# Nine max jobs a head, key copies in the value phase, and the divides on GpSimd in a pooled-attention and Soft-MoE kernel

## The reference

```python
q_pool = q.reshape(B, H, S // 2, 2, D).mean(axis=3)
scores = scale * np.matmul(q_pool, k.transpose(0, 1, 3, 2))
attn = np.exp(scores - np.max(scores, axis=-1, keepdims=True))
attn = attn / (np.sum(attn, axis=-1, keepdims=True) + 1e-09)
x = np.matmul(attn, v)                    # -> (2304, 512)
logits = x @ phi                          # soft MoE: 8 experts, 4 slots each
# softmax over tokens mixes slot inputs, relu(. @ w1) @ w2, softmax over slots mixes back
h = x2 @ w_in                             # then a feed-forward layer, 2048 wide
out = gate(h) @ w_out                     # gate: 0, (h + 1)**2 / 4 or h
```

## Time and profile before

| what | before |
|---|---|
| median of 3 runs (lowest, highest) | 811.72 us (809.96, 811.73) |
| the profiled execution's own time | 812.67 us |
| its span, first to last instruction | 810.8 us |
| busy: PE, DVE, ACT, POOL | 95%, 68%, 59%, 57% |
| attention stage | first exp at 25 us, last sum at 500 us |
| mean granted TensorE clock | 0.989 of full |

### The profile page before, as it was taken

The page is one execution under the profiler, slowest core; times in us unless marked ns, Lnnn a source line. Parts: engine busy times, 40 slices in busy tenths (PEclk is TensorE's granted clock), DMA queues, the critical chain, the costliest instruction groups (busy, mean ns, idle before and its releaser), DMA issues.

```text
span 810.8 us, 14552 instructions
## 1 busy us (share of the span) xinstructions
PE 768.8 (95%) x5181; PEld 575.6 (71%) x5181; DVE 553.2 (68%) x893; ACT 481.1 (59%) x1008; POOL 459.9 (57%) x373
## 2 busy tenths in 40 slices
PE   5899999999999999999999998989799999999996
PEld 3677777776776877777777766524278888888885
DVE  7687887888878878878878873613376454554552
ACT  3677677677676776776776754401565544545452
POOL 2567677677677676676776775000176444444442
PEclk9999999999999999999999999989899999999999
DMA  2222324324334334234243215569900101101011
GB/s 76 78 63 79 103 78 134 99 78 140 94 84 135 94 97 132 83 106 128 78 136 98 79 30 215 196 237 387 387 15 1 40 2 40 27 13 39 0 40 39
DMA packets 47006, 80.63 MB, mean 99 GB/s; under 512 B 9948, under 2 KB 15964, under 8 KB 46940
## 3 DMA queue, kind: packets, MB, share of 16 engines
q1 hardware_dynamic: 46940, 79.77, 31.2%
HBM read 74.89 MB, written 4.79 MB: 98 GB/s over the span
## 4 chain that ended last, share of the span: by engine, by line
PE 46%; POOL 38%; issue 6%; ACT 3%; DVE 3%; DMA 2%; POOLq 0%; SPq 0%; ACTq 0%; DVEq 0%
POOL p_sum L405 33%; PE ps L733 8%; PE ps L732 8%; PE ps L731 8%; POOL p_sum L402 5%; PE ps L490 4%; PE ps L536 3%; ACT probs L796 3%; PE ps L510 2%; PE ps L512 2%; PE ps L721 2%; PE ps L650 2%; DMA w_in<-in_moe_w_in 2%; PE ps L674 1%; PE ps L592 1%
## 5 line engine op out<-in xcount | busy, mean ns | idle before, releaser
L405 POOL TENSOR_TENSOR p_sum<-p_sum,probs 128x576 f32<-128x576 f32 x192 | 271.5, 1414 | 23.2
L1047 DVE TENSOR_REDUCE mx<-ps 128x2 f32<-128x768 f32 (+2 forms) x256 | 216.3, 895 | 23.0 <-PE ps L490 22.9
L796 ACT ACTIVATE probs<-ps 128x576 f32<-128x576 f32 x288 | 184.9, 644 | 38.2 <-PE ps L512 36.5
L510 PE MATMUL ps<-q_rows,k_rows 128*128 128x288 f32 x576 | 172.2, 314 | 0.8 <-ACT probs L796 0.8
L512 PE MATMUL ps<-q_ext,k_ext 128*128 128x288 f32 x576 | 162.2, 296 | 0.0
L439 POOL TENSOR_TENSOR g_lo<-g_buf,g_hi 128x384 fp32r<-128x384 f32 x96 | 100.1, 1043 | 105.3 <-ACT g_hi L952 105.2
L526 PE MATMUL ps<-probs,v_sb 128*64 128x288 f32 x1152 | 146.8, 409 | 1.4 <-ACT probs L796 1.4
L490 PE MATMUL ps<-k_rows,q_rows 128*128 128x384 f32 (+1 forms) x480 | 134.3, 357 | 6.1 <-DVE q_ext L1030 2.9
L510 PEld LDWEIGHTS ps<-q_rows,k_rows 128*128 128x128 f32 x576 | 108.8, 189 | 23.5 <-ACT probs L796 19.6
L1239 DVE SCALAR_TENSOR_TENSOR v_buf<-u_buf 128x384 f32<-128x384 f32 x96 | 58.5, 609 | 92.9 <-ACT u_buf L945 92.7
L526 PEld LDWEIGHTS ps<-probs,v_sb 128*64 128x64 f32 x1152 | 79.9, 137 | 56.2 <-ACT probs L796 1.9
(11 more groups left out here) (170 smaller groups left out, 894.7 us busy)
## 6 DMA issues: line engine op xcount, KB each, us to landing
pre<-in_moe_w SPq DMA_DIRECT2D x47, 512.0 KB, 4.6
k_raw<-in_k SPq DMA_DIRECT2D x32, 288.0 KB, 4.0
v_sb<-in_v SPq DMA_DIRECT2D x32, 288.0 KB, 2.8
q_raw<-in_q SPq DMA_DIRECT2D x32, 256.0 KB, 3.8
from_x<-in_moe_w SPq DMA_DIRECT2D x9, 512.0 KB, 4.5
out<-o_stage SPq DMA_DIRECT2D x36, 128.0 KB, 2.3
p_inv<-inv_dram SPq DMA_DIRECT2D x62, 72.0 KB, 2.6
staged<-in_moe_w SPq DMA_DIRECT2D x8, 512.0 KB, 6.2
```

Source lines behind the costliest of these rows:

```text
L405: nc.gpsimd.tensor_tensor(total, total, probs[u][:, :], ALU.add).then_inc(probs_added, 1)
L510: pe.matmul(ps[:, b0 + h, 0:HALF], k_rows[n % 2][:, P * u:P * u + P], q_rows[n % 2][:, cols], start=True, stop=False)
L796: nc.scalar.activation(probs[u][:, :].rearrange("p (h c) -> p h c", h=2), ps[:, b0:b0 + 2, 0:HALF], ACT.Exp, scale=SCORE_SCALE).then_inc(e ...
L1047: nc.vector.tensor_reduce(mx[0:w, 2 * j:2 * j + len(chunks)], ps[0:w, b:b + len(chunks), 0:CH], AX.X, ALU.max).then_inc(max_free, 1)
```

## The change

Five things change in the attention stage. (1) The half tile's three chunks become three jobs of one chunk each, in banks 6, 7 and 4, so there are nine jobs, the last beside unit 8; its query tile is padded with zeros to 128, and the tiles `q_rows` and `mx` grow. (2) The three key copies of ACT move out of the exps to the value phase, behind the query copies of the same head, two heads ahead. (3) `prepare(n + 2)` stands first in POOL's head. (4) `divide_x` moves from DVE to POOL, behind `prepare` and for head n - 2, with `x_raw` in two buffers and a separate `x_sum` for the sums; DVE keeps head 30's, and the last head's as before. (5) Waits follow from this: ACT's `read_x` on the product two heads back and on the sums' spreading, SP on the last broadcast and on the product before it overwrites `p_inv`, `row_max` and `turn` on other job counts.

```diff
-    JOBS = (CHUNKS + 1) // 2
+    QF = QT - 1
+    PAIR_JOBS = QF * NC // 2
+    JOBS = PAIR_JOBS + NC
@@ job_chunks, job_bank
-            return [(i, i // NC, i % NC) for i in range(2 * j, min(2 * j + 2, CHUNKS))]
+            if j < PAIR_JOBS:
+                return [(i // NC, i % NC) for i in (2 * j, 2 * j + 1)]
+            return [(QF, j - PAIR_JOBS)]
-            return 6 if j % 2 == 0 else 4 if j < JOBS - 1 else 5
+            return (6, 4, 6, 4, 6, 4, 6, 7, 4)[j]
@@ SP: turn_sums
                 sp.wait_ge(sums_inverted, n + 1)
+                if n > 0:
+                    sp.wait_ge(inverses_back, 32 * n)
...
                 sp.wait_ge(inverses_out, 16 * n + 16)
+                if n > 0:
+                    sp.wait_ge(x_done, n)
@@ POOL
+            def divide_x(n):
+                a = D * (n % 2)
+                pool.wait_ge(x_read, n + 1)
+                pool.wait_ge(inverses_back, 32 * n + 32)
+                pool.wait_ge(probs_added, ADDS * (n + 2))
+                pool.wait_ge(q_pooled, min(n + 5, HEADS))
+                nc.gpsimd.tensor_tensor(x_t[a:a + D, n // 2, 0:HALF], x_raw[n % 2][0:D, :], p_inv[0:D, :],
+                                        ALU.mult).then_inc(x_half, 1)
+                pool.wait_ge(x_half, n + 1)
+                nc.gpsimd.tensor_tensor(x_t[a:a + D, n // 2, HALF:SQ], x_raw[n % 2][D:P, :], p_inv[D:P, :],
+                                        ALU.mult).then_inc(x_done, 1)
+                pool.wait_ge(x_done, n + 1)
+
             def head(n):
                 total = p_sum[:, :]
+                if n + 2 < HEADS:
+                    prepare(n + 2)
+                if n > 1:
+                    divide_x(n - 2)
...
-                    if u == 2 and n + 2 < HEADS:
-                        prepare(n + 2)
@@ PE: turn, row_max, weigh
-                        pe.wait_ge(max_free, JOBS * m - 1)
+                        pe.wait_ge(max_free, JOBS * m - 2)
...
+                    if m > 0:
+                        pe.wait_ge(max_free, JOBS * m - 1)
                     pe.wait_ge(q_pooled, m + 1)
...
-                    pe.wait_ge(max_free, JOBS * m + (j - 1))
+                    pe.wait_ge(max_free, JOBS * m + (j - 1 if j < 7 else j - 2))
...
-                    pe.wait_ge(max_free, JOBS * (n + 1) + (JOBS - 2))
+                    pe.wait_ge(max_free, JOBS * (n + 1) + JOBS)
@@ ACT: read_x
+                if n > 1:
+                    act.wait_ge(x_done, n - 1)
                 if n > 0:
-                    act.wait_ge(x_done, n)
+                    act.wait_ge(sums_spread, 16 * n)
@@ ACT: the heads
-                if m == 0:
-                    for j in range(3):
-                        copy_k(0, j)
+                for j in range(3):
+                    copy_k(m, j)
...
                     exp_unit(n, u)
-                    if n + 1 < HEADS and 2 <= u < 5:
-                        copy_k(n + 1, u - 2)
...
                     copy_q(n + 2)
+                    for j in range(3):
+                        copy_k(n + 2, j)
@@ DVE: prologue and heads
+            nc.vector.memset(q_rows[0][:, SQ:QT * P].bitcast(F32), 0.0)
+            nc.vector.memset(q_rows[1][:, SQ:QT * P].bitcast(F32), 0.0)
...
-                if n > 0:
-                    divide_x(n - 1)
+            divide_x(HEADS - 2)
```

More of the change, by code:

```diff
@@ L70, in soft_moe_chain @@
     STEM = 36864
-    AFT = 66176
+    AFT = 67328
     SLOT_AT = 71680
@@ L81, in soft_moe_chain @@
     p_inv = at("p_inv", [P, HALF], 63232)
-    x_raw = at("x_raw", [P, HALF + QUAD], 64384)
+    x_raw = [at("x_raw0", [P, HALF], 64384), at("x_raw1", [P, HALF], 66176)]
+    x_sum = at("x_sum", [P, QUAD], 65536)
     p_spread = at("p_spread", [D, NT], 66112)
@@ L85, in soft_moe_chain @@
     k_ext = [at(f"k_ext{i}", [P, S], AFT + 9216 + 4 * S * i, F32R) for i in range(2)]
[L86 to L91, removed]
+    q_rows = [at(f"q_rows{i}", [P, QT * P], AFT + 18432 + 4 * QT * P * i, F32R) for i in range(2)]
+    q_ext = [at(f"q_ext{i}", [P, QT * P], AFT + 23552 + 4 * QT * P * i, F32R) for i in range(2)]
+    p_sum = at("p_sum", [P, SQ], AFT + 28672)
+    k_raw = at("k_raw", [P, NT, D], AFT + 30976)
+    q_raw = at("q_raw", [P, QT, 2 * D], AFT + 33280)
+    q_pool = at("q_pool", [P, QT, D], AFT + 35840)
     x_nat = at("x_nat", [P, QT, DM], STEM)
@@ L137, in soft_moe_chain @@
     small = {}
-    for name, n in (("ident", P), ("phi_sb", KD * SLOTS), ("sum_ident", SLOTS), ("fold", P), ("mx", 2 * JOBS),
+    for name, n in (("ident", P), ("phi_sb", KD * SLOTS), ("sum_ident", SLOTS), ("fold", P), ("mx", QT * NC),
                     ("neg_max", QT), ("ones", D), ("eps", 1), ("half", 1), ("l_top", 2 * B), ("l_neg", B), ("all_neg", 1),
@@ L169, in soft_moe_chain @@
         scores_ready, exp_done, pv_done = sem("scores_ready"), sem("exp_done"), sem("pv_done")
-        x_read, x_done = sem("x_read"), sem("x_done")
+        x_read, x_half, x_done, x_last = sem("x_read"), sem("x_half"), sem("x_done"), sem("x_last")
         sums_spread, sums_inverted = sem("sums_spread"), sem("sums_inverted")
@@ L297, in turn_sums @@
                 sp.dma_start(p_spread[:, :],
-                             x_raw[0:P:SLOTS, HALF:HALF + QUAD].rearrange("c (p j) -> c p j", j=NT)).then_inc(sums_spread, 16)
+                             x_sum[0:P:SLOTS, :].rearrange("c (p j) -> c p j", j=NT)).then_inc(sums_spread, 16)
                 sp.wait_ge(sums_inverted, n + 1)
+                if n > 0:
+                    sp.wait_ge(inverses_back, 32 * n)
                 sp.dma_start(inv_dram.rearrange("o (p j) -> (o p) j", p=D), p_spread[:, :]).then_inc(inverses_out, 16)
                 sp.wait_ge(inverses_out, 16 * n + 16)
+                if n > 0:
+                    sp.wait_ge(x_done, n)
                 for h in range(2):
@@ L486, in row_max @@
                 else:
-                    pe.wait_ge(max_free, JOBS * m + (j - 1))
-                for b, (i, t, c) in enumerate(job_chunks(j)):
-                    c0, w = q_cols(t)
-                    mm = pe.matmul(ps[0:w, job_bank(j) + b, 0:CH], q_rows[m % 2][:, c0:c0 + w],
+                    pe.wait_ge(max_free, JOBS * m + (j - 1 if j < 7 else j - 2))
+                for b, (t, c) in enumerate(job_chunks(j)):
+                    mm = pe.matmul(ps[:, job_bank(j) + b, 0:CH], q_rows[m % 2][:, P * t:P * t + P],
                                    k_rows[m % 2][:, CH * c:CH * c + CH], start=True, stop=True)
@@ L570, in logits @@
             def logits(b):
-                pe.wait_ge(x_done, 2 * PAIRS * (b + 1))
+                if b < B - 1:
+                    pe.wait_ge(x_done, 2 * PAIRS * (b + 1))
+                else:
+                    pe.wait_ge(x_done, HEADS - 2)
+                    pe.wait_ge(x_last, 2)
                 if b >= 2:
@@ L604, in slot_sums @@
                 if b == 0:
-                    pe.wait_ge(x_done, HEADS)
+                    pe.wait_ge(x_last, 2)
                 else:
@@ L799, in read_x @@
             def read_x(n):
+                if n > 1:
+                    act.wait_ge(x_done, n - 1)
                 if n > 0:
-                    act.wait_ge(x_done, n)
+                    act.wait_ge(sums_spread, 16 * n)
                 act.wait_ge(sums_done, n + 1)
-                nc.scalar.activation(x_raw[:, 0:HALF], ps[:, 4, 0:HALF], ACT.Copy)
-                nc.scalar.activation(x_raw[:, HALF:HALF + QUAD], ps[:, 4, HALF:HALF + QUAD], ACT.Identity,
+                nc.scalar.activation(x_raw[n % 2][:, :], ps[:, 4, 0:HALF], ACT.Copy)
+                nc.scalar.activation(x_sum[:, :], ps[:, 4, HALF:HALF + QUAD], ACT.Identity,
                                      bias=eps[:, :]).then_inc(x_read, 1)
@@ L1043, in top_of_rows @@
             def top_of_rows(m, j):
-                chunks = job_chunks(j)
-                w, b = q_cols(chunks[0][1])[1], job_bank(j)
+                (t, c), n, b = job_chunks(j)[0], len(job_chunks(j)), job_bank(j)
+                w = q_cols(t)[1]
                 dve.wait_ge(max_full, JOBS * m + j + 1)
-                nc.vector.tensor_reduce(mx[0:w, 2 * j:2 * j + len(chunks)], ps[0:w, b:b + len(chunks), 0:CH], AX.X,
+                nc.vector.tensor_reduce(mx[0:w, NC * t + c:NC * t + c + n], ps[0:w, b:b + n, 0:CH], AX.X,
                                         ALU.max).then_inc(max_free, 1)
@@ L1053, in join_tops @@
                     dve.wait_ge(neg_full, m)
-                nc.vector.tensor_reduce(neg_max[:, :], mx[:, 0:CHUNKS].rearrange("p (t c) -> p t c", c=NC), AX.X, ALU.max,
+                nc.vector.tensor_reduce(neg_max[:, :], mx[:, :].rearrange("p (t c) -> p t c", c=NC), AX.X, ALU.max,
                                         negate=True).then_inc(neg_max_ready, 1)
@@ L1072, in divide_x @@
                     last = nc.vector.tensor_tensor(x_t[a:a + D, n // 2, HALF * h:HALF * h + HALF],
-                                                   x_raw[D * h:D * h + D, 0:HALF], p_inv[D * h:D * h + D, :], ALU.mult)
-                last.then_inc(x_done, 1)
```

(4 more changed lines are left out.)

1 line of the change is left out of this document (removed).

## The result

The changed kernel takes 802.13 us (median of 4 runs, 801.74 to 802.85) against 811.73 for the kernel before beside it. The ratio is 0.9888, its 95% interval 0.9871 to 0.9905: faster by 9.6 us, where I had forecast 20.0 and a range that ended at 800. The profiled execution's span is 799.9 us, 10.9 less than before.

A forecast was written before the change was run, and what follows sets the result against it. The prediction took POOL's running sums plus a fixed 3.51 us through PE and ACT as the bound. Span 810.8 - 20.2 + 0.1 = 790.7 us, 792.6 for that run, 0.95 lower for the median: 791.7 us; range 788 to 800.

The forecast's parts named there:

- The binding loop: Attention head: seven POOL additions, one query addition, 3.51 us through PE and ACT; period 14.93 us, falling to 14.25.
- The products' price: Each 64x288 product on POOL, ahead of the next head's first sum: 0.81 us, bounds 0.71 and 1.41.
- rival 1: Slow POOL products overfill the gap: about 815 us at 1.41 us each, extreme about 849 at double DVE's row; 7%.
- the prediction's reading against the Trainium skill: Held that the trace contradicts GpSimd being 2 times slower: POOL 2.45 ns a column, DVE 3.46 for this product.
- it lands 3.9 us later, at 262.65: SP's last query load, issued at 258.75, lands after 3.9 us; taken as landing at 262.35 after the change.
- it fits with 0.4 us left: POOL's query addition and two products end at 265.34, before the next head's first sum is due at 265.74.
- rival 2: Query data come late for POOL's addition; 0.7 us later than taken costs 9 us, about 800 us; 11%.
- 20.2 forecast: Gain in the attention stage from adding query pairs first on POOL: 29 x 0.68 + 0.5 = 20.2 us.
- Price nothing for the key copies: ACT's three copies, 1.62 us, fit in the value phase with 1.0 us left, so cost nothing.
- without any of that gain PE would still have 0.2: Without the 0.45 us from moving the copies, PE would still be ready for column sums 0.2 us before POOL.
- pays nothing by itself: DVE loses two divides of 1.0 us a head, but waited for PE after them anyway (0.56 us): no gain.
- The half tile: Three single maxima jobs for two: DVE 0.2 us later, maxima in time by 0.6 us, priced at nothing.

The follow-up runs named there:

- experiment 3: The changed kernel with the early query load, plus POOL doing the first product twice with the same result; 794.60 us, ratio 0.9787.
- experiment 1: The changed kernel, with SP issuing each head's query load right behind the spreading of the sums instead of behind the key load; 794.86 us, ratio 0.9779.
- experiment 2: The changed kernel, with SP issuing the 512 KB weight piece behind the step's key and query loads instead of ahead; 795.68 us, ratio 0.9794.
- experiment 4: The kernel before with only the query addition moved first in POOL's head; 801.60 us, ratio 0.9852.
- experiment 6: The changed kernel with products back on DVE, and ACT's key copies back between the exps; 800.04 us, ratio 0.9853.
- experiment 8: The changed kernel with products back on DVE, and x_raw in one buffer; 795.20 us, ratio 0.9797.
- experiment 7: The changed kernel with products back on DVE, and the half tile's maxima in two jobs again; 793.87 us, ratio 0.9781.
- experiment 5: The changed kernel with the products back on DVE, everything else of the change kept; 793.43 us, ratio 0.9763.

## Why the prediction was wrong

- **The binding loop** was read rightly: seven sums, the query addition, and a gap through PE and ACT. Taking the addition out of it made the period 14.37 where nothing was late, against 14.25 forecast. Of the 0.12, 0.06 come with the products: with them on DVE the period is 14.31, and the first sum follows ACT's exp after 0.08 us instead of 0.13. The other 0.06 are open.
- **The products' price** was right, 0.80 and 0.81 us for 0.81 forecast, so rival 1 is out; experiment 3 confirms the width of the gap. But the prediction's reading against the Trainium skill (GPSIMD Engine Reference, Engine selection), which puts GpSimd at about twice VectorE's time for such work, was wrong. It compared POOL with DVE's mean of 997 ns, and that is a mean of two unlike products. DVE's product over the whole kernel before (ns: least, median, most):

```profile
L1072 DVE TENSOR_TENSOR x_t<-x_raw,p_inv x62: 453/1116/1573, 52.6 to 495.5; 64x288 f32<-64x288 f32 x62
```

  In most heads the first product of the two overlaps POOL's last sum and takes 1.54 us, and the second runs while POOL is idle and takes 0.45. POOL's 0.80 is 1.8 times that, so the trace agrees with the page after all. What rival 1 had wrong was to double the slowed row.
- **The step that failed** is "it lands 3.9 us later, at 262.65", and with it "it fits with 0.4 us left". The issue was forecast well, 3.8 us ahead of the sums' end, and so it came in most heads. The landing was mis-sized in two ways. A median of four loads stood for a duration that ran up to 5.9 us in the same trace; and the 32 KB load became slower, from a median of 3.8 us to 4.3, for a reason that is open (the weight piece is ahead of it in both kernels). A head's loss is not symmetric: early data gain nothing, late data cost their excess, so the spread decides, not the median. In the 29 periods the gap could absorb a landing some 0.7 us behind the sums' end (0.5 by the prediction's figures), and 12 loads came later, up to 2.3 us behind it. By an estimate of mine, the loads of the kernel before, each landing taken relative to its sums' end and moved later by the 0.36 us between 4.16 and 3.8 us of issue, would have cost some 6 us of lateness; so most of the loss could be read before. I had this as rival 2 with 11% and a price of 9 us at 0.7 us of lateness, about 800. Measured were 7.8 us of lateness. Experiments 1 and 2 show the cause.
- **Where the 20.0 went:** 9.6 were seen. The early load gives back 7.3 us by medians (8.9 by ratios), and 29 x 0.12 = 3.5 us are the longer undisturbed period. That is 20.4 to 22.0 against 20.0. The traces of the attention stage say the same: 8.6 us gained, 7.8 lost to late data, 0.7 to the longer idling, 3.5 to the period, 20.6 in all for 20.2 forecast.
- **Price nothing for the key copies** was right for ACT, and wrong in what I said of PE: "without any of that gain PE would still have 0.2". I had taken PE's reserve from the weight loads' wait, 0.88 us. The products' own wait for the same sums, in the kernel before, is the row that counts:

```profile
PE ps L536 <- POOL p_sum L405: 8.5, 23, 0.4
```

  That is 0.37 us a head, so without the copies' move PE should bind at 14.93 - 0.37 = 14.56. Two experiments without it agree: 14.50 with eight jobs (experiment 4) and 14.55 with nine (experiment 6). Whether the 0.05 between them is the ninth job's was not tested.
- **DVE's relief "pays nothing by itself"** was right, and keeping the products on DVE costs nothing but in the 3 to 6 periods in which a single `x_raw` meets a slowed second product (experiments 4 and 8). The copies' move is what lifted PE's bound from 14.55 to below 14.31; the second buffer only took away those few periods.
- **The half tile** was priced at nothing, and experiment 7 measured nothing.

## What to carry to other kernels

When work is moved to the front of a wait that it must fit into, look for the longest value over the whole run of whatever releases it, not for the median of one stretch; a load that was harmless in mid-queue becomes the release of the chain, and what is queued just ahead of it counts. Take a TensorE reserve from the wait of its products, not from that of its weight loads. And undo a change part by part: here one part gave the gain, two made room for it (the copies' move is worth 6.6 us, the second buffer 1.8), one did nothing, and the one that looked like relief for a busy engine cost 8.7 us (802.13 against 793.43), most of it by using up the slack: with early data it costs 1.4. Last, look at more than one head before naming what binds: in experiment 4 most heads and the six long ones had different bounds.

## What was not expected of the hardware

- The same 32 KB load took between 2.6 and 6.0 us to land in the changed kernel. Issued behind a 512 KB piece the median was 4.3 us, with the piece behind the loads 3.8, and far from other loads 2.5.
- A 64x288 product with two inputs took 0.45 us on DVE while POOL was idle, and 1.03 to 1.17 us where POOL's addition had started just ahead of it. It works the other way too: POOL's query addition took 1.12 us instead of 0.87 where DVE's product had started 0.06 us ahead of it.
- Some 187 us apart (periods ending at 71, 258 and 445 us in experiment 1) one period is 0.3 to 0.4 us longer than the others. POOL idles there between two running sums, 0.51, 0.43 and 0.43 us instead of 0.14. In the three kernels that have two products a head on POOL (the changed one and experiments 1 and 2) it strikes the same heads, 13 apart, although the times differ; the kernel before and experiment 5 show none. What interrupts there is open; no run was made for it.
